# Two-pass products with v, a doubled output buffer and MLP groups dealt in halves in a fused attention and MLP kernel

## The chip, the cores and the metric

The kernel runs on one core of a Trainium2 chip. Its time is device microseconds for one execution of the whole program.

## What is computed

Four batches of 8 heads of causal (in blocks of 64) attention over 576 positions with head dimension 64, then an MLP (512 to 2048 to 512, leaky ReLU), then a routed mixture of eight experts. All in float32 precision: operands are split into a high part, which TensorE's fp32r format holds, and a low rest, and a product is made of high x high, high x low and low x high.

```python
    scores = scale * np.matmul(q, k.transpose(0, 1, 3, 2))
    mask = block_i >= block_j
    scores = np.where(mask, scores, -1000000000.0)
    scores = scores - np.max(scores, axis=-1, keepdims=True)
    attn = np.exp(scores)
    attn = attn / (np.sum(attn, axis=-1, keepdims=True) + 1e-09)
    return np.matmul(attn, v).astype(np.float32)
...
    h = x @ w_in
    g = np.maximum(0.01 * h, h)
    return (g @ w_out).astype(np.float32)
```

The experts come after everything that the change touches.

## The kernel before

Heads are worked in 16 pairs of two. A pair has nine units, numbered i = 0 to 8: rows of queries in tiles of 128, four for the even head (i = 0 to 3), one that holds the last 64 rows of both heads (i = 4, TAIL), four for the odd head (i = 5 to 8). Unit u = 9p + i goes through: scores on TensorE (line 1219), maximum on VectorE (955), exponential on ScalarE (812, with the row's sum), transposes of the probabilities on TensorE (1251) into one of two PSUM banks of ps_t, then high part pt_hi on ScalarE (822) and low part pt_lo on VectorE (963). All engines run the same loop over steps s = 0 to 155, each with its own lag and in strict order: in step s TensorE does scores(s + 2), transposes(s - 2), products with v by the table P_V, then MLP groups by the table FILL; VectorE does maximum(s), low_p(s - 3); ScalarE does high_p(s - 3), exponential(s), then copies of MLP results of step s - 1.

The product with v of a pair (p_v, 1265) accumulates both heads in one bank, ps_o: v stands between zero columns, so that the even head fills rows 0 to 63 and the odd one 64 to 127. Per head there are two kinds: half 0 (query columns 0 to 255; two tiles of keys, six products) and half 1 (columns 256 to 575; five tiles, fifteen products of 320, 192 and 64 columns, dealt as eight in step 3 or 5 and seven in step 4 or 6). VectorE copies each half out of PSUM once (copy_o, 983), GpSimd multiplies it with the spread inverse of the row sums (normalise, 657), and from it come xh and xl, the MLP's input. v is rounded to v_hi on ScalarE (high_v, 802) and v_lo is made on GpSimd (low_v, 647). The row sums get their epsilon and are inverted on VectorE (invert, 968), turned on TensorE (turn_inverse, 1291) into ps_o, copied and spread through DRAM by SyncE.

An MLP group (hidden, 1295) is twelve products of 384 columns into one bank (ps_h1), and ScalarE copies it out (copy_hidden, 835; line 839 issues it). There are 96, of which 64 are dealt into the steps by fill_steps (76): groups 0 to 15 over steps 50 to 83, 16 to 47 over 86 to 119, 48 to 56 over 122 to 143, each whole at the end of a step; from group 57 on there are two banks and one group a step. w_in's 16 pieces are rounded on ScalarE (high_w_in, 830) every second step from 42 and completed on GpSimd. After step 155 the rest of the MLP and the experts follow.

## Time and profile before

| | us |
|---|---|
| median of 3 runs | 856.89 (856.85 to 856.97) |
| the profiled execution | 856.37 |
| its span | 854.5 |
| TensorE / VectorE / ScalarE / GpSimd busy | 810.5 / 414.2 / 359.7 / 196.8 |
| mean granted TensorE clock | 0.98 of 2.4 GHz |

Busy time is a share of the span over stages of different kind. An instruction's duration on TensorE overlaps the next one's, so what it costs is read from start to start. "Idle before" in brackets is how long the engine had nothing running before an instruction, with what ended that. The granted clock is the mean of a stretch over two levels, 2.4 GHz (1.0) and 1.2 GHz (0.5).

### The profile page before, as it was taken

The numbers are of one execution on the slowest core, as the hardware profiler recorded it, in microseconds if no ns is written. First come the engines' busy times: TensorE is split into PE (matmuls) and PEld (weight loads), VectorE is DVE, ScalarE is ACT, GpSimd is POOL, SyncE is SP. The second block draws the span as 40 slices with busy tenths as digits, with TensorE's granted clock in tenths as the row PEclk, the third lists the DMA queues.
The fourth block names the chain that finished last, engine by engine and source line by source line (L and its number), as shares of the span: only waits on it lengthen the run. The fifth ranks groups of instructions, "written<-read, shape, count | busy, mean of one in ns | idle before, by whom it ended". The sixth has DMA issues, their size and how long they took to land.

```text
span 854.5 us, 14147 instructions
## 1 busy us (share of the span) xinstructions
PE 810.5 (95%) x4885; PEld 736.9 (86%) x4885; DVE 414.2 (48%) x835; ACT 359.7 (42%) x850; POOL 196.8 (23%) x226
## 2 busy tenths in 40 slices
PE   4889999999999999999999999999999589999999
PEld 3778899999999999899998888888888489888887
DVE  4777766664334456402335455555553232344464
ACT  4677767665445566423442222221221031333353
POOL 5354666433213224110010000000000141221221
PEclk9999799999999999999999999999999879999999
DMA  6444466744453343136666655655561137577740
GB/s 149 132 122 136 142 186 195 203 126 141 118 146 112 105 137 105 50 98 193 173 180 182 190 148 172 182 180 145 168 186 50 38 113 248 174 216 233 227 135 3
DMA packets 101545, 126.82 MB, mean 148 GB/s; under 512 B 15986, under 2 KB 62210, under 8 KB 101480
## 3 DMA queue, kind: packets, MB, share of 16 engines
q1 hardware_dynamic: 98392, 121.33, 48.3%
q0 software_dynamic: 2000, 3.77, 1.4%
q10 hardware_dynamic: 1088, 0.89, 0.5%
q8 instruction: 37, 0.61, 0.3%
q14 instruction: 28, 0.23, 0.1%
HBM read 92.58 MB, written 31.57 MB: 145 GB/s over the span
## 4 chain that ended last, share of the span: by engine, by line
PE 89%; DVE 4%; issue 3%; ACT 3%; DMA 1%; POOL 0%; SPq 0%; DVEq 0%; ACTq 0%; POOLq 0%
PE ps_hid L1431 11%; PE ps_o L1286 9%; PE ps_h L1310 8%; PE ps_x L1345 8%; PE ps_x L1347 8%; PE ps_h L1312 8%; PE ps_h L1311 8%; PE ps_x L1346 8%; PE ps_t L1262 4%; PE ps_y L1442 3%; PE ps_y L1443 3%; PE ps_y L1444 3%; PE ps_s L1247 2%; PE ps_s L1248 2%; PE ps_s L1237 1%
## 5 line engine op out<-in xcount | busy, mean ns | idle before, releaser
L966 DVE TENSOR_TENSOR pt_lo<-ps_t,pt_hi 128x512 fp32r<-128x512 f32 (+4 forms) x160 | 76.5, 486 | 147.1 <-ACT pt_hi L828 146.8
L1310 PE MATMUL ps_h<-xh,win_h 128*128 128x384 f32 x384 | 132.8, 346 | 1.3 <-ACT act L839 1.0
L1311 PE MATMUL ps_h<-xl,win_h 128*128 128x384 f32 x384 | 128.8, 335 | 0.0
L1312 PE MATMUL ps_h<-xh,win_l 128*128 128x384 f32 x384 | 128.7, 335 | 0.0
L1345 PE MATMUL ps_x<-wout_h,g_hi 128*128 128x512 f32 x288 | 116.3, 404 | 0.0
L1347 PE MATMUL ps_x<-wout_h,g_lo 128*128 128x512 f32 x288 | 112.9, 392 | 0.0
L1346 PE MATMUL ps_x<-wout_l,g_hi 128*128 128x512 f32 x288 | 112.1, 389 | 0.0
L1431 PEld LDWEIGHTS ps_hid<-rows_t,w_sb 128*128 128x128 f32 x768 | 89.5, 196 | 8.8 <-issue 8.4
L1431 PE MATMUL ps_hid<-rows_t,w_sb 128*128 128x128 f32 x768 | 91.0, 281 | 5.1 <-PE ps_y L1444 4.2
L839 ACT ACTIVATE act<-ps_h 128x384 f32<-128x384 f32 x96 | 47.1, 491 | 110.1 <-PE ps_h L1312 108.4
L819 ACT ACTIVATE prob<-ps_s,neg_max 128x128 f32<-128x128 f32 (+2 forms) x144 | 78.9, 548 | 25.7 <-DVE neg_max L960 25.2
L828 ACT ACTIVATE pt_hi<-ps_t 128x512 fp32r<-128x512 f32 (+4 forms) x160 | 67.6, 434 | 50.3 <-PE ps_o L1286 31.4
L643 POOL TENSOR_TENSOR k_st<-k_raw,k_st 64x576 fp32r<-64x576 f32 x32 | 45.9, 1433 | 161.6 <-DVE k_st L946 151.1
L1262 PE MATMUL ps_t<-ident,prob 128*128 128x128 f32 x384 | 70.5, 288 | 5.3 <-DVE pt_lo L966 5.3
L1310 PEld LDWEIGHTS ps_h<-xh,win_h 128*128 128x128 f32 x384 | 72.1, 188 | 3.8 <-ACT act L839 1.7
L1003 DVE TENSOR_TENSOR g_lo<-g_raw,g_hi 128x512 fp32r<-128x512 f32 x72 | 49.5, 687 | 52.2 <-ACT g_hi L849 52.2
L960 DVE TENSOR_REDUCE neg_max<-ps_s 128x1 f32<-128x128 f32 (+2 forms) x144 | 72.4, 503 | 0.6 <-PE ps_s L1248 0.5
L1286 PE MATMUL ps_o<-pt_hi,v_hi 128*128 128x320 f32 (+3 forms) x224 | 69.6, 311 | 2.7 <-DVE o_f L988 2.7
L1311 PEld LDWEIGHTS ps_h<-xl,win_h 128*128 128x128 f32 x384 | 72.2, 188 | 0.0
L1312 PEld LDWEIGHTS ps_h<-xh,win_l 128*128 128x128 f32 x384 | 72.1, 188 | 0.0
L1286 PE MATMUL ps_o<-pt_hi,v_lo 128*128 128x320 f32 (+3 forms) x224 | 68.6, 306 | 0.0
L1286 PE MATMUL ps_o<-pt_lo,v_hi 128*128 128x320 f32 (+3 forms) x224 | 66.1, 295 | 0.0
(154 smaller groups left out, 1422.3 us busy)
## 6 DMA issues: line engine op xcount, KB each, us to landing
w_sb<-in_w SPq DMA_DIRECT2D x64, 512.0 KB, 5.2
hidden<-act SPq DMA_DIRECT2D x96, 192.0 KB, 2.2
g_raw<-hidden SPq DMA_DIRECT2D x72, 256.0 KB, 4.5
k_raw<-in_k_t SPq DMA_DIRECT2D x62, 144.0 KB, 2.9
q_raw<-in_q_t SPq DMA_DIRECT2D x32, 144.0 KB, 2.9
x2rows<-x SPq DMA_DIRECT2D x18, 256.0 KB, 2.4
out<-x SPq DMA_DIRECT2D x18, 256.0 KB, 2.6
k<-k_st SPq DMA_DIRECT2D x31, 144.0 KB, 2.7
```

The costliest lines, as they stand in the source:

```text
L819: e.activation(prob_of(u), score_out(u), ACT.Exp, bias=neg_max[:, u % 4:u % 4 + 1], scale=1.0, accum_out=row_sum[p % 2][:, i:i + 1]).then_ ...
L960: e.tensor_reduce(out=neg_max[:, u % 4:u % 4 + 1], in_=src, axis=AX.XY if u % UNITS == TAIL else AX.X, op=ALU.max, negate=True).then_inc(s ...
L966: e.tensor_tensor(lo, src, hi.bitcast(F32), ALU.subtract).then_inc(s_ptlo, 1)
L1262: last = e.transpose(t_bank(u, P, P * kt, P * kt + P), tile[:, P * kt:P * kt + P], ident[:, :])
L1286: last = e.matmul(ps_o[:, a:a + cols], stat, (pt_hi, pt_lo, pt_hi)[j][0:kr, h, at:at + cols], start=h == 0 and n == 0, stop=h == 1 and n = ...
L1310: e.matmul(dst, win_h[:, f, kc, :], xh[slot][:, kc, :], start=kc == 0, stop=False)
L1311: e.matmul(dst, win_h[:, f, kc, :], xl[slot][:, kc, :], start=False, stop=False)
L1312: last = e.matmul(dst, win_l[:, f, kc, :], xh[slot][:, kc, :], start=False, stop=kc == KC - 1)
L1345: e.matmul(dst, hi, wout_h[:, f, :], start=f == 0, stop=False)
L1346: e.matmul(dst, hi, wout_l[:, f, :], start=False, stop=False)
L1347: last = e.matmul(dst, lo, wout_h[:, f, :], start=False, stop=f == FC - 1)
L1431: last = e.matmul(ps_hid[half][:, P * f - HALF * half:P * (f + 1) - HALF * half], w1_sb[i][:, c, P * f:P * f + P], rows_t[:, c, :], start= ...
```

## The change

- Products with v: the stationary operand now holds high and low part of v side by side (v_st, four slots), so one pass with pt_hi and one with pt_lo give high rows and low rows at once; each head has its own high and low rows. The last 64 keys take one pass: v is loaded twice, into both halves of the partitions, and pt_lo of these keys goes into the lower half of pt_hi's tile. Four products for half 0, nine for half 1, in steps 7, 1, 3, 5. Three rounds of the bank: both heads' half 0 side by side, then half 1 of each head.
- Getting them out: ScalarE copies the low rows (copy_low, 4 per pair, steps 2, 2, 4, 6), VectorE adds them to the high rows (add_o), o_f has two buffers.
- Moves: v's and w_in's rounding to VectorE, the epsilon to ScalarE; v's load to step 4; low_v, low_x, normalise, low_q and copy_inverse to other steps; the inverse is turned into a bank of the transposes.
- A third bank (the MLP's, ps_h1) for transposes up to unit 44.
- MLP groups are issued in two halves of six products. The deal goes by halves up to group 56; a result is copied in the step after its second half. By the formula steps 50 to 83 and 122 to 143 hold at most one half each, steps 86 to 119 one or two: both of one group in 86 to 93 and 103 to 110, and the second of one with the first of the next in 95 to 101 and 112 to 118.

The diff, cut:

```diff
 STEPS = N_UNITS + 12
-P_V = {8: (0, 0, 0, 6), 1: (1, 0, 0, 6), 3: (0, 1, 0, 8), 4: (0, 1, 8, 15), 5: (1, 1, 0, 8), 6: (1, 1, 8, 15)}
+P_V = {7: (0, 0), 1: (1, 0), 3: (0, 1), 5: (1, 1)}
+V_EVEN, V_EVEN_LOW, V_ODD_LOW, V_ODD = range(4)
+V_SLOTS = 4
 MASKED = -float(1 << 30)
...
     for g in range(N_ATT_HID):
-        if g < FC:
-            at[50 + 34 * g // FC].append(g)
-        elif g < 3 * FC:
-            at[86 + 34 * (g - FC) // (2 * FC)].append(g)
-        elif g < TWO_BANKS:
-            at[122 + 5 * (g - 3 * FC) // 2].append(g)
-        else:
-            at[N_UNITS + 5 + g - TWO_BANKS].append(g)
+        for part in range(2):
+            n = 2 * g + part
+            if g < FC:
+                s = 50 + 34 * n // (2 * FC)
+            elif g < 3 * FC:
+                s = 86 + 34 * (n - 2 * FC) // (4 * FC)
+            elif g < TWO_BANKS:
+                s = 122 + 22 * (n - 6 * FC) // (2 * (TWO_BANKS - 3 * FC))
+            else:
+                s = N_UNITS + 5 + g - TWO_BANKS
+            at[s].append((g, part))
     return at
+def filled_at(s):
...
+    return u % 3 if u < T3_UNITS else u % 2
+def t_before(u):
+    return next((v for v in range(u - 1, max(u - 4, -1), -1) if t_index(v) == t_index(u)), None)
...
-            c = BANK * (u % 2)
-            return ps_t[0:rows_, c + a:c + z]
+            n = t_index(u)
+            return ps_h1[0:rows_, a:z] if n == 2 else ps_t[0:rows_, BANK * n + a:BANK * n + z]
...
                 return views
             src = t_bank(u, P, 0, P * (qt + 1)).rearrange("p (k q) -> p k q", q=P)
             return [[src] + [t[:, h, PT_B:PT_W].rearrange("p (k c) -> p k c", k=4)[:, 0:qt + 1, P * (qt - 2):P * (qt - 1)]
                              for t in (pt_hi, pt_lo)]]
...
-                e.wait_ge(s_vlo, 2 * p)
+                e.wait_ge(s_vlo, p)
             e.dma_start(v_raw[:, 0:QT - 1, :],
                         v_r[b, 0:full, hp * P:(hp + 1) * P].rearrange("(t p) c -> p t c", p=P)).then_inc(s_v, 16)
...
+                e.dma_start(v_raw[half:half + D, QT - 1, :], v_r[b, full:S, hp * P:(hp + 1) * P]).then_inc(s_v, 16)
...
                         copy_k(2 * p + 2)
+                    if i == 4 and p + 1 < N_PAIRS:
+                        load_v(e, p + 1)
...
-                    e.tensor_tensor(v_lo[i][0:rows_, t0:t1, 0:3:2, :],
-                                    v_raw[0:rows_, t0:t1, :].rearrange("p t (g c) -> p t g c", g=2),
-                                    v_hi[i][0:rows_, t0:t1, 0:3:2, :].bitcast(F32), ALU.subtract).then_inc(s_vlo, 1)
+                e.wait_ge(*before[0])
+                e.wait_ge(s_vhi, p + 1)
+                before[0] = s_vlo, p + 1
+                e.tensor_tensor(v_st[i][:, :, V_EVEN_LOW:V_ODD_LOW + 1, :],
+                                v_raw[:, :, :].rearrange("p t (g c) -> p t g c", g=2),
+                                v_st[i][:, :, V_EVEN:V_ODD + 1:V_ODD - V_EVEN, :].bitcast(F32),
+                                ALU.subtract).then_inc(s_vlo, 1)
...
                     if i == 7:
                         low_k(2 * p + 3)
-                if i == 2 and 1 <= p < N_PAIRS:
+                if i == 7 and 1 <= p <= N_PAIRS:
+                    normalise(p - 1)
+                if i == 1 and p < N_PAIRS:
                     low_v(p)
-                if i == 8 and 1 <= p <= N_PAIRS:
-                    normalise(p - 1)
-                if i == 1 and 2 <= p <= N_PAIRS + 1:
+                if i == 2 and 2 <= p <= N_PAIRS + 1:
                     low_x(p - 2)
                 f, odd = divmod(s - 42, 2)
...
+                rs = row_sum[p % 2]
+                e.wait_ge(s_exp, UNITS * (p + 1))
+                e.activation(rs[:, :], rs[:, :], ACT.Copy, bias=1e-9).then_inc(s_eps, 1)
+            def copy_low(p, h, half):
+                n = product(p, h, half)
+                cols = B_COLS if half else A_COLS
+                own, low = head_rows(h)
+                e.wait_ge(s_pv, n + 2 - h if half == 0 else n + 1)
+                if n >= 2:
+                    e.wait_ge(s_of, n - 1)
+                at = A_COLS * h if half == 0 else 0
+                e.activation(o_low[own, 0:cols], ps_o[low, at:at + cols], ACT.Copy).then_inc(s_olow, 1)
...
                 for src, hi, _ in pt_views(u):
...
-                    if i == 8:
-                        high_v(p + 1)
                     if i == 7:
                         high_q(2 * p + 3)
+                if i == 8 and p < N_PAIRS:
+                    add_epsilon(p)
+                if 1 <= p <= N_PAIRS:
+                    if i == 2:
+                        copy_low(p - 1, 0, 0)
+                        copy_low(p - 1, 1, 0)
+                    if i == 4:
+                        copy_low(p - 1, 0, 1)
+                    if i == 6:
+                        copy_low(p - 1, 1, 1)
                 if i == 0 and 2 <= p <= N_PAIRS + 1:
                     high_x(p - 2)
...
-                e.wait_ge(s_exp, UNITS * (p + 1))
-                e.tensor_scalar(rs[:, :], rs[:, :], 1e-9, None, ALU.add).then_inc(s_eps, 1)
...
-                e.reciprocal(inv[:, :], rs[:, :]).then_inc(s_inv, 1)
...
+                e.tensor_copy(inv_t[:, :], t_bank(UNITS * (p + 1), UNITS, 2 * P, 3 * P)).then_inc(s_invt, 1)
...
                 a, z = ((0, A_COLS), (A_COLS, S))[half]
-                e.wait_ge(s_pv, 4 * p + 2 * half + 2)
-                if p >= 1:
-                    e.wait_ge(s_norm, p)
-                e.tensor_copy(o_f[:, a:z], ps_o[:, 0:z - a]).then_inc(s_of, 1)
+                own, _ = head_rows(h)
+                n = product(p, h, half)
+                e.wait_ge(s_olow, n + 2 - h if half == 0 else n + 1)
+                if p >= 2:
+                    e.wait_ge(s_norm, p - 1)
+                at = A_COLS * h if half == 0 else 0
+                e.tensor_tensor(o_f[p % 2][own, a:z], ps_o[own, at:at + z - a], o_low[own, 0:z - a], ALU.add).then_inc(s_of, 1)
+            def high_v(p):
+                e.wait_ge(s_v, 48 * (p + 1))
+                if p >= 2:
+                    e.wait_ge(s_pv, 4 * (p - 1))
+                e.tensor_copy(v_st[p % 2][:, :, V_EVEN:V_ODD + 1:V_ODD - V_EVEN, :],
+                              v_raw[:, :, :].rearrange("p t (g c) -> p t g c", g=2)).then_inc(s_vhi, 1)
+            def high_w_in(f):
+                e.wait_ge(s_stage[f % 2], 16 * (f // 2 + 1))
+                e.tensor_copy(win_h[:, f, :, :], w_stage[f % 2][:, :].rearrange("p (k c) -> p k c", k=KC)).then_inc(s_winh, 1)
             def low_w_out(f):
...
                     low_q(2 * p + 1)
                 if i == 0 and 1 <= p <= N_PAIRS:
                     invert(p - 1)
-                if i == 2 and 1 <= p <= N_PAIRS:
+                if i == 3 and 1 <= p <= N_PAIRS:
                     copy_inverse(p - 1)
-                    copy_o(p - 1, 0)
-                if i == 7 and 1 <= p <= N_PAIRS:
-                    copy_o(p - 1, 1)
+                if 1 <= p <= N_PAIRS:
+                    if i == 2:
+                        add_o(p - 1, 0, 0)
+                        add_o(p - 1, 1, 0)
+                    if i == 4:
+                        add_o(p - 1, 0, 1)
+                    if i == 6:
+                        add_o(p - 1, 1, 1)
+                if i == 0 and p < N_PAIRS:
+                    high_v(p)
+                f, odd = divmod(s - 42, 2)
+                if odd == 0 and 0 <= f < FC:
+                    high_w_in(f)
...
-                i = u % UNITS
+                v, i = t_before(u), u % UNITS
+                if v is not None:
+                    e.wait_ge(s_ptlo, split_done(v))
+                    if v >= UNITS and v % UNITS == 0:
+                        e.wait_ge(s_invt, v // UNITS)
...
+            def p_v(p, h, half):
+                n = product(p, h, half)
+                e.wait_ge(s_ptlo, split_done(UNITS * p + (1, TAIL + 1, TAIL + 2, UNITS - 1)[2 * h + half]))
+                if n % 4 == 0:
+                    e.wait_ge(s_vlo, p + 1)
+                if n % 4 != 1 and n >= 2:
+                    e.wait_ge(s_of, n)
+                at_o = A_COLS * h if half == 0 else 0
+                v = v_st[p % 2]
+                steps = [(kt, low) for kt in range(4 if half else 2) for low in range(2)]
+                if half:
+                    steps.append((QT - 1, 0))
+                for kt, low in steps:
...
+                last.then_inc(s_pv, 1)
...
                 slot = m % 4
+                dst = ps_hidden(g)
+                if part == 0:
+                    hidden_waits(g)
+                for kc in range(KC // 2 * part, KC // 2 * (part + 1)):
+                    e.matmul(dst, win_h[:, f, kc, :], xh[slot][:, kc, :], start=kc == 0, stop=False)
+                    e.matmul(dst, win_h[:, f, kc, :], xl[slot][:, kc, :], start=False, stop=False)
+                    last = e.matmul(dst, win_l[:, f, kc, :], xh[slot][:, kc, :], start=False, stop=kc == KC - 1)
+                if part:
+                    last.then_inc(s_h, 1)
+            def hidden_waits(g):
+                m, f = divmod(g, FC)
+                if g == 0:
+                    e.wait_ge(s_ptlo, split_done(T3_UNITS - 1))
                 if f == 0:
                     e.wait_ge(s_xlo, x_ready(m))
...
                     e.wait_ge(s_act, g)
-                dst = ps_hidden(g)
-                for kc in range(KC):
-                    e.matmul(dst, win_h[:, f, kc, :], xh[slot][:, kc, :], start=kc == 0, stop=False)
-                    e.matmul(dst, win_h[:, f, kc, :], xl[slot][:, kc, :], start=False, stop=False)
-                    last = e.matmul(dst, win_l[:, f, kc, :], xh[slot][:, kc, :], start=False, stop=kc == KC - 1)
-                last.then_inc(s_h, 1)
             scores(0)
             scores(1)
             for s in range(STEPS):
                 if s + 2 < N_UNITS:
                     scores(s + 2)
+                p, i = divmod(s, UNITS)
+                if i == 2 and 1 <= p <= N_PAIRS:
+                    turn_inverse(p - 1)
                 if 2 <= s < N_UNITS + 2:
                     transposes(s - 2)
...
+                for part in range(2):
+                    hidden(g, part)
```

## Rows read from the trace of the kernel before

**Rows 1.** The page, part 1: busy us, share of the span, instructions of each engine.
```profile
PE 810.5 (95%) x4885; PEld 736.9 (86%) x4885; DVE 414.2 (48%) x835; ACT 359.7 (42%) x850; POOL 196.8 (23%) x226
```

**Rows 2.** Busy time by stage: stretch, length, busy (instructions) of each engine, granted clock.
```profile
26.50:104.70 78.20, 68.62 (x422) 60.44 (x421) 57.57 (x128) 54.02 (x158) 39.46 (x35) 0.89 0.46 130
104.70:185.50 80.80, 80.24 (x542) 77.53 (x540) 50.04 (x108) 56.25 (x159) 45.84 (x39) 1.00 0.64 181
...
188.50:303.90 115.40, 114.67 (x732) 110.88 (x730) 49.29 (x107) 59.16 (x163) 29.44 (x27) 1.00 0.43 125
...
59.80:76.50 16.70, 14.91 (x95) 13.25 (x94) 12.44 (x28) 11.60 (x36) 7.63 (x8) 0.91 0.44 126
...
136.70:156.90 20.20, 20.20 (x139) 19.59 (x139) 12.98 (x28) 15.17 (x44) 13.44 (x11) 1.00 0.58 176
...
200.10:231.90 31.80, 31.62 (x203) 30.62 (x202) 12.83 (x28) 16.05 (x45) 7.71 (x7) 1.00 0.43 123
```

**Rows 3.** Timeline of TensorE in a filled pair: start us, duration us, engine, line, operation.
```profile
128.22 0.39 PE L1286 MATMUL ps_o<-pt_hi,v_hi 128*128 128x320 f32 x1
...
129.47 0.39 PE L1247 MATMUL ps_s<-k_st,q_hi 128*128 128x512 f32 x1
...
130.29 0.39 PE L1286 MATMUL ps_o<-pt_hi,v_lo 128*128 128x320 f32 x1
130.52 0.25 PE L1286 MATMUL ps_o<-pt_hi,v_hi 128*128 128x192 f32 x1
...
130.93 0.29 PE L1286 MATMUL ps_o<-pt_hi,v_hi 64*128 64x64 f32 x1
...
131.38 0.44 PE L1310 MATMUL ps_h<-xh,win_h 128*128 128x384 f32 x1
131.66 0.34 PE L1311 MATMUL ps_h<-xl,win_h 128*128 128x384 f32 x1
131.83 0.35 PE L1312 MATMUL ps_h<-xh,win_l 128*128 128x384 f32 x1
...
138.72 0.36 PE L1286 MATMUL ps_o<-pt_hi,v_hi 128*128 128x256 f32 x1
...
139.44 0.27 PE L1293 MATMUL ps_o<-ident,inv 128*9 128x128 f32 x1
```

**Rows 4.** The same timeline with ScalarE: one MLP group's end to the next one's start.
```profile
202.23 0.33 PE L1312 MATMUL ps_h<-xh,win_l 128*128 128x384 f32 x1
...
202.60 0.49 ACT L839 ACTIVATE act<-ps_h 128x384 f32<-128x384 f32 x1 [1.38 <-PE ps_h L1312]
...
203.14 0.44 PE L1310 MATMUL ps_h<-xh,win_h 128*128 128x384 f32 x1
```

**Rows 5.** Instructions by line: count, shortest, median and longest ns.
```profile
L988 DVE COPY o_f<-ps_o x32: 402/440/491, 31.0 to 366.9; 128x256 f32<-128x256 f32 x16, 128x320 f32<-128x320 f32 x16
...
L946 DVE CAST k_st<-k_raw x32: 437/450/1102, 7.8 to 333.7; 128x576 fp32r<-128x576 f32 x32
...
L971 DVE TENSOR_SCALAR row_sum<-row_sum x16: 156/764/979, 28.1 to 357.3; 128x9 f32<-128x9 f32 x16
...
L828 ACT ACTIVATE pt_hi<-ps_t x160: 258/428/604, 16.3 to 358.2; 128x512 fp32r<-128x512 f32 x48, 128x128 fp32r<-128x128 f32 x32, 128x256 fp32r<-128x256 f32 x32, 128x384 fp32r<-128x384 f32 x32
...
L808 ACT ACTIVATE v_hi<-v_raw x32: 293/462/627, 12.3 to 336.6; 128x512 fp32r<-128x512 f32 x16, 64x128 fp32r<-64x128 f32 x16
```

**Rows 6.** VectorE's timeline, 43 to 60 us, idle in brackets; and waits, 43.1 to 93.7.
```profile
51.95 0.56 DVE L966 TENSOR_TENSOR pt_lo<-ps_t,pt_hi 128x384 fp32r<-128x384 f32 x1 [0.86 <-ACT pt_hi L828]
...
56.03 0.69 DVE L966 TENSOR_TENSOR pt_lo<-ps_t,pt_hi 128x512 fp32r<-128x512 f32 x1 [1.40 <-ACT pt_hi L828]
...
59.92 0.42 DVE L966 TENSOR_TENSOR pt_lo<-ps_t,pt_hi 128x256 fp32r<-128x256 f32 x1 [1.25 <-ACT pt_hi L828]
...
PE ps_t L1262 <- DVE pt_lo L966: 3.0, 4, 0.8
```

**Rows 7.** Busy time by stage, the end of the stretch without filler, units 45 to 49.
```profile
93.70:104.70 11.00, 9.99 (x50) 8.93 (x49) 7.87 (x16) 7.20 (x22) 9.07 (x8) 0.62 0.39 120
```

107 lines of the change are left out of this document (34 added, 73 removed).

## The prediction

> **What bounds the kernel now.** I read the page first: TensorE is busy 95% of the span, VectorE 48%, ScalarE 42% [rows 1]. An average hides stages, so next came busy time by stage, cut where the exponentials (line 819, one per unit, nine units per pair of heads) of units 9, 50, 86, 120 and 143 start [rows 2]. Three kinds of stretch show. From 104.7 to 355.5 us MLP groups fill TensorE and it has 0.6 and 0.7 us idle in stages of 81 and 115 us: there every product less is time less. From 26.5 to 104.7 no MLP work exists, TensorE is idle 9.6 of 78.2 us, its granted clock averages 0.89, and no engine is full: waits between engines set the pace, 16.7 us a pair. Everything after 372 us is untouched. Last I read TensorE's timeline for what a product costs from start to start (durations overlap, so they overstate it) [rows 3, 4], and VectorE's waits in a pair without filler [rows 6].
>
> **1. Products with v.** Each head had 6 + 15 products and gets 4 + 9. Of the second kind, the first part of 8 took 129.47 - 128.22 = 1.25 us, the other 7 took 131.38 - 130.29 = 1.09. The first product after transposes costs 0.23 (130.29 to 130.52), each later one of 320 columns (1.25 - 0.23)/7 = 0.146; three of 192 stand between 130.52 and 130.93; the three with 64 rows take 0.45 [rows 3]. New: 0.23 + 5 x 0.146 + 0.20 (two of 192, a step of 0.1 each without the 64-row product behind them) + 0.11 (one of 64 columns, now over 128 rows: a little above the step of 192 columns, below the 0.15 of a 64-row one) = 1.27, so 2.34 - 1.27 = 1.07 saved. First kind: six took 139.44 - 138.72 = 0.72; 0.08 of it is the entry (0.23 - 0.146), and four of six leave 0.08 + 0.43 = 0.51, so 0.21 saved. Per head 1.28, **per pair 2.6 us**. Bounds for that 128-row product: 0.05 and 0.20, 0.2 us a pair at most.
>
> **2. Halving the MLP groups.** Two things follow from the new deal. (a) Entering a group costs 131.66 - 131.38 = 0.28 against 0.17 inside it (131.83 - 131.66) [rows 3]: 0.1 us per extra entry. Groups 0 to 15 and 48 to 56 are split over two steps: 25 extra entries, 2.5 us. (b) In steps 95 to 101 and 112 to 118 the formula puts the second half of group g and the first half of g + 1 in one step, 14 times. Both use one PSUM bank, so the later half waits until ScalarE has copied g. The trace has that handover at its shortest: last product starts 202.23, copy 202.60 to 203.09, next group's first product 203.14 [rows 4]. That is 0.91 against 0.17 back to back, **0.74 us** of idle TensorE; in the kernel before, scores and transposes lay in this gap, now nothing does. 14 x 0.74 = 10.4 us. ScalarE issues that copy after the next step's pt_hi, exponential and whatever else the step holds. Where that is a q_hi (0.6), a pair of xh (0.7) or two new copies (0.7), the copy comes some 0.5 us later: 7 of the 14 steps, 3.8 us with small change. Bounds of (b): 10.4 and 18.
>
> **3. Halves of the output.** Products leave high and low rows apart, so ScalarE copies one half (4 per pair) and VectorE adds (4 per pair, instead of 2 copies). No such form is in the trace; nearest are the copies of the same columns on VectorE, median 0.44, and ScalarE's pt_hi from PSUM, median 0.43 [rows 5]. Neighbouring instructions overlap by a little under 0.1, so 1.4 us more for ScalarE, 0.8 for VectorE per pair. Bounds per instruction 0.3 and 0.6. The adds stand in VectorE's queue in front of the next maximum, and behind a ScalarE copy: in step 2 TensorE's next product waits for exp, two copies and two adds, where it waited for two copies of VectorE. I take 0.9 us a pair for this where there is no filler, and nothing where TensorE lags behind the others anyway. Bounds 0 and 2.
>
> **4. Moves between engines.** v's rounding (two instructions of 0.29 to 0.63 on ScalarE) and w_in's (16 of about 0.6) go to VectorE, where a cast of 128x576 has a median of 0.45; the epsilon (median 0.76 on VectorE) goes to ScalarE, estimated at 0.2 from pt_hi's shortest, 0.26 [rows 5]. Per pair VectorE: -0.9 + 0.45 + 0.8 = +0.35, and 4.5 x 0.45 = 2.0 in the pairs with w_in; ScalarE: -0.7 + 0.15 + 1.4 = +0.85. In the shortest filled pair VectorE goes from 13.0 to 15.4 of then some 18 us, ScalarE stays at 15 or below [rows 2]: covered by TensorE, VectorE narrowly. The epsilon shows a danger: nine columns took from 0.16 to 0.98 us, and the cast reached 1.10 [rows 5]. The Trainium skill (SBUF — State Buffer, Who interferes with whom) says the same of such pairs: a VectorE copy in a two-port mode and a GpSimd instruction exclude each other for a whole instruction. The trace agrees in kind with the 0.98; by the rule each of the 32 new casts might gain that delay. A median close to the cast's shortest (0.45, 0.44) says that it is rare, and the sum goes by that.
> GpSimd: one v_lo instead of two, low x a step later (needed three steps later), normalising a step earlier; it is busy 13.4 of 20.2 us at most [rows 2]. SyncE: v's load moves from step 2 to 4 and gets a third DMA; behind it stand the spreading of the inverse at step 5 and the hidden stores; its wait (v_lo of step 1) has long been met. On ScalarE's queue the third DMA stands ahead of the first table load at the start, while four memsets leave GpSimd: I take 0, between -1 and +2 (two fewer or four more instructions of v_hi's 0.46 on that path). The turned inverse shares a transpose bank and holds the transposes of unit 2 until VectorE's step 3 ends: bounds 0 and 0.7 a pair without filler, in the value below.
>
> **5. The stretch without filler.** VectorE is busy 12.4 of 16.7 us and idles 4.3 [rows 2], 3.5 of it in three waits for pt_hi, 0.86, 1.40 and 1.25 us [rows 6]. The first two end when a product lump of step 4 or 6 is done, as its pt_hi may not overwrite what the product reads; the lumps now end in steps 3 and 5. The third follows v_hi (0.7) on ScalarE, now gone. The third bank takes TensorE's wait for pt_lo (3.0 us in three pairs) [rows 6]. So of 4.3 the three waits go but for 0.1, and 1.4 come (0.9 of point 3, 0.5 for the inverse and the later adds): 2.3 idle and 12.4 + 0.35 busy make 15.05, **1.65 saved a pair**. Bounds: no idle at all (12.7) and nothing saved.
>
> **The sum** against the profiled 856.4 (span 854.5 and 1.9 around it; the median of the runs is 0.5 higher):
> - 0 to 26.5: 0.
> - 26.5 to 104.7, 4.7 pairs: -7.8.
> - 104.7 to 185.5, units 50 to 83, 3.8 pairs: -9.8, +1.6 (16 entries), +1.5 (where the next half follows a short step, up to 0.3 of the 0.91 shows): -6.7.
> - 185.5 to 188.5, one product group: -1.
> - 188.5 to 303.9, 3.8 pairs: -9.8 + 10.4 + 3.8 = **+4.4**. This stage gets slower.
> - 303.9 to 355.5, 2.7 pairs: -7.0 + 0.9 + 0.7 = -5.4.
> - 355.5 to 372: -2.4, +0.9 for adds with nothing beside them: -1.5.
> Together -18.0: 838.4, as a median **838.9**.
>
> **Rivals.**
> A. *The halves cost nothing* (0.12): the bank handover is hidden and the second filled stage gives its 9.8. For it: in the kernel before nearly every copy lay beside other products. Against: the copy's end and the next product stand 0.05 apart [rows 4]. -18.0 - 14.2: 824.7.
> B. *The new copy and add bind* (0.12): without filler nothing is gained, and the first filled stage loses another 3 us as VectorE, with its w_in casts, makes TensorE wait. For it: VectorE has 50.0 of 80.8 us there already [rows 2], and waits stand in strict queues. Against: TensorE saturated. -18.0 + 7.8 + 3: 849.7.
> C. *TensorE's clock stays low* (0.06), the slower side. The granted clock is 0.89 over the stretch without filler [rows 2], a fifth of it at the lower level, and 0.62 over its end [rows 7]. Less product work makes the engine quieter. Its work in a pair: 31.8 us [rows 2] less 8.5 groups of 12 x 0.173 + 0.1 = 2.18 is 13.3, then 10.7. All at 1.2 GHz it is 21.4 instead of 16.7: +22 over 4.7 pairs, 838.9 + 7.8 + 22 = 869. It makes the whole slower once a pair takes 18.8, that is with three quarters of the stretch at the low level; now it is a fifth. Against: at the low level the same work keeps TensorE busy, and it came back each time. The Trainium skill (TensorE: Matmul & The Clock Gate, The HAM clock gate) has the same two levels and says that activity releases the throttle; it speaks for a swing, not for staying low.
>
> **How the numbers follow.** Forecast 0.70, A 0.12, B 0.12, C 0.06. The forecast's own range, from the bounds of points 2, 3 and 5 that don't all fall together, is 830 to 847; to hold 8 in 10 it is widened to 827 to 850, which takes in B and part of A's near side. This kernel's runs tell 0.2% (1.7 us) from no change. Faster: all but C and an edge of B, 0.92; same 0.02; slower 0.06.
>
> **What would show it.** Step 1: 416 products at ps_o instead of 672, starts 0.146 apart. Step 2: 14 idle times of 0.7 to 1.3 us before the first MLP product, ended by ScalarE's act, and units 86 to 119 taking 118 to 122 us instead of 115.4. Step 3: TensorE waiting for o_f in step 3 of pairs without filler. Step 5: 15 us between pairs' first exponentials. Wrong would be: units 86 to 119 below 112 us (A), pairs of 16.5 without filler (B), a clock below 0.75 before unit 50 (C).

## The result and the profile after

The changed kernel takes 865.1 us (median of 4 runs, 863.95 to 866.94) against 856.9 for the kernel before on the same chip: ratio 1.009, 95% interval 1.007 to 1.011. It is 0.9% slower, where 838.9 was forecast. Its profiled execution took 864.9 us, with a span of 863.1; the kernel before had 854.5.

The page of the changed kernel: busy time, share of the span and instructions of each engine, then the first product of the MLP groups (busy, mean ns, idle before it and what ended that).

```profile
PE 784.2 (91%) x4629; PEld 705.8 (82%) x4629; DVE 445.6 (52%) x883; ACT 370.9 (43%) x882; POOL 194.0 (22%) x206
...
L1357 PE MATMUL ps_h<-xh,win_h 128*128 128x384 f32 x384 | 137.8, 359 | 20.9 <-ACT act L866 20.6
```

TensorE has 256 matmuls fewer and 26.3 us less busy time than in [rows 1], and the kernel is 8.6 us longer: TensorE's idle time went from 44.0 to 78.9 us. Of that, 20.6 stand at the first product of an MLP group and wait for ScalarE's copy of the group before.

Busy time by stage (stretch, length, busy and instructions of TensorE, its weight loads, VectorE, ScalarE, GpSimd, then granted clock, DMA share, GB/s), cut where [rows 2] is cut; the second row ends 3.6 us before unit 86, and the last is one pair without filler:

```profile
25.90:109.70 83.80, 61.45 (x349) 53.46 (x347) 66.52 (x143) 58.58 (x168) 39.00 (x30) 0.84 0.45 126
109.70:190.20 80.50, 73.95 (x480) 69.90 (x481) 61.49 (x127) 55.15 (x157) 45.62 (x35) 1.00 0.65 181
...
193.80:313.00 119.20, 107.67 (x661) 100.52 (x662) 53.52 (x113) 62.13 (x171) 29.25 (x23) 1.00 0.44 121
313.00:361.80 48.80, 45.62 (x307) 43.42 (x306) 34.34 (x74) 35.52 (x102) 17.12 (x13) 1.00 0.39 106
361.80:388.30 26.50, 22.62 (x122) 22.00 (x121) 4.34 (x11) 8.51 (x21) 4.54 (x5) 0.87 0.20 62
...
78.50:97.20 18.70, 13.98 (x78) 12.65 (x77) 14.92 (x33) 12.96 (x39) 9.30 (x8) 0.78 0.53 150
```

Set against the forecast, with the stages named by the exponentials that bound them (us; "miss" is measured less forecast):

| stage | before | after | measured | forecast | miss |
|---|---|---|---|---|---|
| start to unit 9 | 26.5 | 25.9 | -0.6 | 0 | -0.6 |
| units 9 to 49, no filler | 78.2 | 83.8 | +5.6 | -7.8 | +13.4 |
| units 50 to 85 | 83.9 | 84.0 | +0.1 | -7.7 | +7.8 |
| units 86 to 119 | 115.3 | 119.3 | +4.0 | +4.4 | -0.4 |
| units 120 to 142 | 51.6 | 48.8 | -2.8 | -5.4 | +2.6 |
| 143 to the first MLP group after attention | 23.9 | 26.5 | +2.6 | -1.5 | +4.1 |
| the rest | 475.1 | 474.8 | -0.3 | 0 | -0.3 |

So the third row of loss was foreseen and the first, the largest, was not: half of the miss lies where there is no MLP work.

Next the waits of that stretch, 26 to 105 us of the kernel before and 26 to 110 of the changed one (engine, line, what it waited for: total us, times, longest). Before:

```profile
DVE pt_lo L966 <- ACT pt_hi L828: 20.1, 23, 1.8
...
PE ps_t L1262 <- DVE pt_lo L966: 4.0, 6, 0.8
...
PE ps_s L1237 <- ACT prob L819: 3.4, 5, 0.7
```

After:

```profile
PE ps_s L1288 <- DVE q L981: 13.5, 5, 2.7
DVE o_f L1018 <- ACT o_low L842: 10.7, 14, 1.0
...
DVE pt_lo L996 <- ACT pt_hi L860: 6.0, 13, 0.8
```

The waits that the forecast removed did go: VectorE's for pt_hi fell from 20.1 to 6.0 us, TensorE's for pt_lo is not in the list. In their place TensorE stands still once a pair, 2.7 us, before the scores of step 2 (line 1288), and VectorE waits at the adds. The timeline around one such place (start, duration, engine, line, operation, idle before it in brackets):

```profile
60.74 1.42 POOL L688 TENSOR_TENSOR inv_all<-o_f,inv_all 128x576 f32<-128x576 f32 x1
...
61.54 0.76 DVE L1024 CAST v_st<-v_raw 128x640 fp32r<-128x640 f32 x1
...
62.19 0.78 ACT L826 ACTIVATE xh<-inv_all 128x384 fp32r<-128x384 f32 x2 [0.80 <-POOL inv_all L688]
...
62.88 0.47 ACT L860 ACTIVATE pt_hi<-ps_t 128x384 fp32r<-128x384 f32 x1
...
63.38 0.56 DVE L996 TENSOR_TENSOR pt_lo<-ps_t,pt_hi 128x384 fp32r<-128x384 f32 x1 [0.75 <-ACT pt_hi L860]
...
63.85 0.81 DVE L981 SCALAR_TENSOR_TENSOR q<-q_raw,q_hi 64x640 fp32r<-64x640 f32 x1
...
64.91 1.18 PE L1288 MATMUL ps_s<-k_st,q_hi 128*128 128x288 f32 x4 [2.68 <-DVE q L981]
```

Read backwards: the scores wait for q, q stands in VectorE's queue behind pt_lo, pt_lo waits for pt_hi, pt_hi stands in ScalarE's queue behind xh, and xh waits for GpSimd's normalise. VectorE's own casts stand in the same chain. Which link carries the time a timeline can't say; the experiments had to.

### The profile page after: what moved, and what is told of

The parts are those of the page before. It is cut to its first block, busy times and chain, and to the rows that moved or that the text cites. A ratio compares the mean times of both kernels' runs of the same rounds, so it can differ in the third digit from the quotient of the medians.

```text
span 863.1 us, 13813 instructions
## 1 busy us (share of the span) xinstructions
PE 784.2 (91%) x4629; PEld 705.8 (82%) x4629; DVE 445.6 (52%) x883; ACT 370.9 (43%) x882; POOL 194.0 (22%) x206
## 4 chain that ended last, share of the span: by engine, by line
PE 76%; ACT 7%; issue 6%; DVE 6%; POOL 2%; DMA 1%; SPq 1%; ACTq 1%; DVEq 0%; POOLq 0%
PE ps_hid L1495 10%; PE ps_x L1409 8%; PE ps_x L1411 8%; PE ps_x L1410 8%; PE ps_h L1357 7%; PE ps_h L1359 6%; PE ps_h L1358 6%; PE ps_o L1339 3%; PE ps_t L1315 3%; PE ps_y L1506 3%; PE ps_y L1507 3%; PE ps_y L1508 3%; ACT prob L851 2%; DVE neg_max L990 2%; DVE q L981 2%
## 5 line engine op out<-in xcount | busy, mean ns | idle before, releaser
L1357 PE MATMUL ps_h<-xh,win_h 128*128 128x384 f32 x384 | 137.8, 359 | 20.9 <-ACT act L866 20.6
L996 DVE TENSOR_TENSOR pt_lo<-ps_t,pt_hi 128x128 fp32r<-128x128 f32 (+2 forms) x129 | 65.8, 510 | 90.4 <-ACT pt_hi L860 89.7
L860 ACT ACTIVATE pt_hi<-ps_t 128x512 fp32r<-128x512 f32 (+4 forms) x140 | 60.0, 437 | 62.4 <-PE ps_t L1315 61.7
L670 POOL TENSOR_TENSOR k_st<-k_raw,k_st 64x576 fp32r<-64x576 f32 x32 | 46.3, 1446 | 162.5 <-DVE k_st L976 162.5
L1339 PE MATMUL ps_o<-pt_hi,v_st 128*128 128x320 f32 (+3 forms) x224 | 65.3, 310 | 5.4 <-DVE o_f L1018 5.3
L876 ACT ACTIVATE g_hi<-g_raw 128x512 fp32r<-128x512 f32 x72 | 43.6, 627 | 50.6 <-DVE g_raw L1039 42.7
L1298 PE MATMUL ps_s<-k_st,q_hi 128*128 128x128 f32 (+3 forms) x128 | 47.2, 369 | 18.7 <-POOL ident L708 10.6
L1411 PEld LDWEIGHTS ps_x<-wout_h,g_lo 128*128 128x128 f32 x288 | 54.0, 188 | 12.1
```

What stands on the lines that cost most here:

```text
L860: e.activation(hi, src, ACT.Copy).then_inc(s_pthi, 1)
L996: e.tensor_tensor(lo, src, hi.bitcast(F32), ALU.subtract).then_inc(s_ptlo, 1)
L1339: last = e.matmul(ps_o[:, at_o + a:at_o + a + cols], v[:, kt, 2 * h:2 * h + 2, :].rearrange("p g c -> p (g c)"), (pt_lo if low else pt_hi) ...
L1357: e.matmul(dst, win_h[:, f, kc, :], xh[slot][:, kc, :], start=kc == 0, stop=False)
L1411: last = e.matmul(dst, lo, wout_h[:, f, :], start=False, stop=f == FC - 1)
```

## The experiments

Stage lengths of all of them (us, same marks; the last column is the median with the ratio to the kernel before on the same chip). Each profile is one execution; a step under about 1 us is not read. The ratio is to the kernel before in the same set of runs, whose median was 856.9 in the first and 858.5 to 859.4 in the later ones, so medians of different sets differ by up to 2 us for that alone.

| kernel | 9 to 49 | 50 to 85 | 86 to 119 | 120 to 142 | median, ratio |
|---|---|---|---|---|---|
| before | 78.2 | 83.9 | 115.3 | 51.6 | 856.9 |
| after | 83.8 | 84.0 | 119.3 | 48.8 | 865.1, 1.009 |
| e1 | 82.3 | 82.8 | 119.3 | 48.8 | 862.9, 1.005 |
| e2 | 84.0 | 84.2 | 106.0 | 48.5 | 851.3, 0.991 |
| e3 | 78.1 | 89.8 | 127.7 | 56.6 | 881.7, 1.027 |
| e4 | 82.0 | 80.5 | 106.0 | 46.2 | 845.0, 0.984 |
| e5 | 79.9 | 81.5 | 106.0 | 46.7 | 844.2, 0.982 |
| e6 | 80.3 | 79.3 | 106.0 | 46.7 | 841.8, 0.979 |
| e7 | 76.7 | 77.3 | 106.6 | 44.5 | 835.0, 0.972 |
| e8 | 81.9 | 81.0 | 106.0 | 46.2 | 845.1, 0.983 |
| e9 | 83.6 | 80.4 | 106.0 | 47.3 | 847.2, 0.988 |
| e10 | 80.0 | 80.9 | 106.1 | 46.6 | 841.4, 0.980 |
| e11 | 84.2 | 81.1 | 106.0 | 47.7 | 845.2, 0.984 |
| e12 | 84.3 | 85.9 | 113.1 | 49.7 | 862.1, 1.006 |
| e13 | 74.1 | 77.4 | 106.6 | 46.4 | 833.3, 0.971 |
| e14 | 78.4 | 78.5 | 106.3 | 46.3 | 837.6, 0.976 |

**e1: the second low_q back in step 0.** The wait in the timeline above names q, and the change moved it a step later.

```diff
-                if i == 1 and 1 <= p < N_PAIRS:
+                if i == 0 and 1 <= p < N_PAIRS:
                     low_q(2 * p + 1)
```

> The changed kernel with one line moved back: VectorE's low part of the odd head's q is made in step 0 again, ahead of the inverse and of v's rounding, instead of at the end of step 1. Theory 1 (TensorE's wait of 2.7 us per pair before the scores of unit 4 is the wait for this instruction, and it also brings the clock down): pairs without filler fall from 17.5 to about 15.5 us, units 9 to 49 from 83.8 to about 74 us, the whole to about 854. Rival (the same engine has the same work, so the wait only moves to the maxima and exponentials behind it): pairs stay within 0.5 us of 17.5, the whole within 2 us of 865.

Measured 862.9 us, the stage 82.3: 1.5 us of 5.6. Most of the wait is still there, 10.7 of 13.5 us over the stretch, under another name; around one place:

```profile
59.93 1.43 POOL L688 TENSOR_TENSOR inv_all<-o_f,inv_all 128x576 f32<-128x576 f32 x1
...
60.60 1.43 DVE L981 SCALAR_TENSOR_TENSOR q<-q_raw,q_hi 64x640 fp32r<-64x640 f32 x1
...
62.08 0.75 DVE L1024 CAST v_st<-v_raw 128x640 fp32r<-128x640 f32 x1
62.76 0.40 DVE L990 TENSOR_REDUCE neg_max<-ps_s 128x1 f32<-128x256 f32 x1
...
63.20 0.47 ACT L851 ACTIVATE prob<-ps_s,neg_max 128x256 f32<-128x256 f32 x1 [0.66 <-DVE neg_max L990]
...
63.91 1.20 PE L1288 MATMUL ps_s<-k_st,q_hi 128*128 128x288 f32 x4 [2.48 <-ACT prob L851]
```

The scores of step 2 take two of the ring's four banks at once; they now wait for the exponential that frees the second, it for the maximum, and that for v's cast and for q, which beside GpSimd's normalise took 1.43 us instead of 0.81. The move alone is a small part of the loss.

**e2: MLP groups of units 86 to 119 whole again.**

```diff
             elif g < 3 * FC:
-                s = 86 + 34 * (n - 2 * FC) // (4 * FC)
+                s = 86 + 34 * (g - FC) // (2 * FC)
```

> The changed kernel with groups 16 to 47 dealt whole again, one per step, so that no step holds the second half of one group and the first of the next; all else as changed. Theory (each of the 14 handovers of the bank costs TensorE 0.74 us and more): units 86 to 119 fall from 119.3 to about 105 us and the whole to about 851. Rival A (the handovers are covered, TensorE is short of other things): less than 4 us.

Measured 851.3 us. The stage falls from 119.3 to 106.0 us and TensorE is busy 105.5 of it; no other stage moves by more than 0.3. The waits at a group's first product, in this stage of the changed kernel and of e2:

```profile
PEld ps_h L1357 <- ACT act L866: 16.6, 17, 1.5
...
PE ps_h L1357 <- ACT act L866: 11.2, 14, 1.2
```

```profile
PEld ps_h L1357 <- ACT act L866: 1.9, 6, 0.4
```

Fourteen waits of the product: the number of shared steps is the one that the formula gives. They are 11.2 us of idle time, 0.80 each; TensorE's busy time in the stage is 2.2 us longer as well (107.7 against 105.5). Together that is 13.3 us, 0.95 for each place, between the two bounds of the forecast.

**e3: the kernel before with its MLP groups in halves, and nothing else.** Its deal is the changed kernel's, with twice as many issues of six products.

```diff
-                for g in FILL[s]:
-                    hidden(g)
+                for g, part in FILL[s]:
+                    hidden(g, part)
```

> The kernel before with the changed kernel's deal of half groups and nothing else. Theory: 14 x 0.74 to 1.0 = 10 to 14 us more in units 86 to 119 (115.3 to 126 or above), 0.1 us for each of 25 more entries elsewhere, the whole 868 to 874. Rival (the deal in halves smooths the steps and gains where a whole group made engines wait): units 50 to 85 and 120 to 142 get shorter by more than 1 us each.

Measured 881.7 us, 1.027 of the kernel before, above the 868 to 874 that were expected. Nothing changes before unit 50; then +5.9, +12.4 and +5.0 us. In units 50 to 85 no step holds parts of two groups. TensorE is busy 84.2 of 89.8 us there, where the kernel before had 83.3 of 83.9: 5.0 of the 5.9 us are idle time. That is 0.37 for each of the 16 groups split. The waits of that stage:

```profile
PEld ps_h L1310 <- issue: 5.5, 5, 1.7
PE ps_h L1310 <- ACT act L847: 4.5, 4, 1.5
...
PE ps_h L1310 <- POOL win_l L684: 1.0, 1, 1.0
```

Five waits of 5.5 us carry it, four of them for the copy. The second half of one group stands at the end of its step and the first half of the next in the following one; where little lies between, the bank is not free. Halves cost in all three filled stages, and the forecast had seen nearly all of the price in the middle one.

**e4: both together (q's step and whole groups everywhere).** The rest of the change stays.

```diff
-                s = 50 + 34 * n // (2 * FC)
+                s = 50 + 34 * g // FC
...
-                s = 122 + 22 * (n - 6 * FC) // (2 * (TWO_BANKS - 3 * FC))
+                s = 122 + 5 * (g - 3 * FC) // 2
```

> The changed kernel with low q back in step 0 and all groups dealt whole, as in the kernel before. If the two causes are separate, the gains add: units 9 to 49 about 74 us, units 86 to 119 about 105 us, the whole about 838 to 842. If VectorE and ScalarE then bind in units 50 to 85, that stage stays at 80 us or above and the whole near 845.

Measured 845.0 us, 0.984. Against the kernel before, the middle stage gives 9.3 us, close to the 9.8 of point 1; but units 50 to 85 give 3.4 instead of 9.8, and the stretch without filler still loses 3.8. It is the base of what follows.

**e12: the products' work as before, on e4's base.** Three passes instead of two and three of the last keys' part, pt_hi's pass counted twice.

```diff
-                steps = [(kt, low) for kt in range(4 if half else 2) for low in range(2)]
+                steps = [(kt, low) for kt in range(4 if half else 2) for low in (0, 1, 0)]
                 if half:
-                    steps.append((QT - 1, 0))
+                    steps += [(QT - 1, 0)] * 3
```

> As the kernel with low q in step 0 and whole groups (844.95 us), with the products with v issued three times per tile as in the kernel before (21 per head instead of 13; the output is not right, one pass is counted twice). It shows where the saved products count. Theory: in the filled stages their whole time, 3.8 x 2.5 = 9.5 us in units 86 to 119 and less in 50 to 85, where VectorE binds; in the stretch without filler nothing to 1 us a pair, because no chain there runs through them. Rival (they count everywhere): units 9 to 49 up by 4.7 x 2.5 = 12 us.

Measured 862.1 us. It puts back 7.1 us in units 86 to 119 (the other 2.2 of e4's 9.3 come with the rest of the change, such as fewer pieces of a product and the last keys over 128 rows, which no run parts), 5.4 in units 50 to 85, and only 2.3 in the stretch without filler, 0.5 a pair. By the middle stage's price, 7.1 over 3.8 pairs, it would be 8.8: where there is no filler, three quarters of the products' work lies beside waits. This splits the stretch's balance: the rest of the change costs 84.3 - 78.2 = 6.1 us there, the products return 2.3. In units 50 to 85 the rest costs 2.0 (85.9 against 83.9).

**e5 and e6: the roundings back on ScalarE**, v's first, then w_in's too (two functions moved, on e4).

```diff
-                if i == 0 and p < N_PAIRS:
-                    high_v(p)
...
+                if i == 8 and p + 1 < N_PAIRS:
+                    high_v(p + 1)
...
+                e.activation(v_st[p % 2][:, :, V_EVEN:V_ODD + 1:V_ODD - V_EVEN, :],
+                             v_raw[:, :, :].rearrange("p t (g c) -> p t g c", g=2), ACT.Copy).then_inc(s_vhi, 1)
```

> As the kernel with low q in step 0 and whole groups (844.95 us), with v's rounding back on ScalarE at the end of step 8 instead of VectorE's step 0. Theory 2 (without filler the chain runs through VectorE's steps 0 and 1: q, inverse, v's rounding, maximum, then ScalarE's exponential and the scores of unit 4): 0.5 to 0.7 us of the chain goes, pairs without filler fall from 17.3 to 16.6 us or below, units 9 to 49 from 82.0 to about 79 us, the whole to about 841. Rival (ScalarE gets the same delay in the same place, in front of the same exponential): no change within 1 us.

> The same with w_in's rounding back on ScalarE too. Theory 3 (in units 50 to 85 VectorE, busy 64 of 80.5 us, binds instead of TensorE): 16 instructions of 0.45 us leave it and that stage falls from 80.5 to 76 or 77 us, what TensorE's saved products would give; the whole to about 837. Rival (ScalarE becomes the bound there): 79 us or more.

Measured 844.2 and 841.8 us. Both expectations asked for more, 841 and 837. v's rounding is worth 2.1 us in the stretch without filler, of which 1.0 is lost again in units 50 to 85, and the intervals of e4's and e5's ratios overlap; w_in's is worth 2.2 in units 50 to 85. VectorE's busy time in the stretch fell by 6.4 us (68.3 to 62.0) for 1.7 us of time: its load alone does not set the pace. ScalarE took the work over, so this does not say what less work would bring.

**e7: no low rows.** The copies of the low rows are left out and the adds are copies of the high rows of the same size, so the output lacks the low rows' part.

```diff
-                e.wait_ge(s_olow, n + 2 - h if half == 0 else n + 1)
+                e.wait_ge(s_pv, n + 2 - h if half == 0 else n + 1)
...
-                e.tensor_tensor(o_f[p % 2][own, a:z], ps_o[own, at:at + z - a], o_low[own, 0:z - a], ALU.add).then_inc(s_of, 1)
+                e.tensor_copy(o_f[p % 2][own, a:z], ps_o[own, at:at + z - a]).then_inc(s_of, 1)
```

> As the kernel with low q in step 0 and whole groups (844.95 us), but the low rows are left out: ScalarE doesn't copy them and VectorE copies the high rows alone, four times per pair, so the part of the output from v's low rows is missing. It prices the handover from TensorE by ScalarE to VectorE. Theory 4 (VectorE's queue stands at each add until ScalarE has copied, 8 us in units 9 to 49, and the products of the next step wait for the add): units 9 to 49 fall from 82.0 to about 75 us, units 50 to 85 from 80.5 to about 77, the whole to about 833. Rival (the waits are slack): less than 2 us in either stage.

Measured 835.0 us: -5.3 in the stretch, -3.2 in units 50 to 85. The handover from ScalarE to VectorE is the largest single part found. The two stages, e4 and then e7:

```profile
25.80:107.80 82.00, 62.89 (x349) 55.74 (x348) 68.34 (x143) 58.77 (x168) 38.20 (x30) 0.79 0.46 129
107.80:188.30 80.50, 75.48 (x497) 71.54 (x497) 64.12 (x133) 58.08 (x164) 47.20 (x36) 1.00 0.66 188
```

```profile
26.00:102.70 76.70, 60.24 (x343) 54.30 (x342) 67.83 (x142) 50.50 (x149) 37.37 (x30) 0.80 0.48 134
102.70:180.10 77.40, 74.62 (x498) 71.52 (x499) 62.67 (x132) 51.71 (x150) 47.69 (x37) 1.00 0.69 197
```

VectorE has as much to do as in e4, and ScalarE 8.3 us less in the first stage. The gain is that of ScalarE's copies and of VectorE standing still for them; this run can't part the two.

**e8: two banks for the transposes**, as before.

```diff
-T3_UNITS = 5 * UNITS
+T3_UNITS = 0
```

> As the kernel with low q in step 0 and whole groups (844.95 us), with two banks for the transposes throughout instead of three up to unit 44. If the third bank carries something, the 1 us per pair that transposes waited for pt_lo before comes back: units 9 to 49 from 82.0 to 84 or 86 us. If VectorE and ScalarE set the pace there, no more than 1 us.

Measured 845.1 us against 845.0, the stretch 81.9 against 82.0. The third bank is worth nothing on this base.

**e9: GpSimd normalises before it takes the low part of k**, on e6's base. The timeline of after shows xh waiting 0.80 us for the normalise.

```diff
-                    if i == 7:
-                        low_k(2 * p + 3)
                 if i == 7 and 1 <= p <= N_PAIRS:
                     normalise(p - 1)
+                if p + 1 < N_PAIRS:
+                    if i == 7:
+                        low_k(2 * p + 3)
```

> As the kernel with low q in step 0, whole groups and both roundings on ScalarE (841.75 us), with GpSimd's step 7 turned round: it normalises first and makes the low part of k after it. Theory 5 (there the chain of a pair without filler runs k's cast, low k, normalise, xh, pt_hi: GpSimd's two instructions of 1.4 us stand in it one behind the other, while GpSimd idled 6 us before): pairs without filler fall from 16.9 to about 15.5 us, units 9 to 49 from 80.3 to 74 us, the whole to about 835. Rival (the adds and exponentials set the same pace by themselves): less than 2 us.

Measured 847.2 us against e6's 841.8, the stretch 83.6 against 80.3. The theory falls. There was little left to gain: in e6 the waits of xh for the normalise are 0.5 us over the stretch, none above 0.2, where the changed kernel has 3.0. And the multiply now begins beside VectorE's cast of k, and that cast took 1.67 us for a median of 0.45. The low part of k begins at 60.40, later by the multiply's 1.41 us and by 0.46 more for the cast; which of the two costs the 3.3 us no run parts:

```profile
58.53 1.41 POOL L688 TENSOR_TENSOR inv_all<-o_f,inv_all 128x576 f32<-128x576 f32 x1 [5.65 <-DMA inv_all<-inverse]
...
58.58 1.67 DVE L996 CAST k_st<-k_raw 128x576 fp32r<-128x576 f32 x1
...
60.40 1.40 POOL L670 TENSOR_TENSOR k_st<-k_raw,k_st 64x576 fp32r<-64x576 f32 x1 [0.46 <-DVE k_st L996]
```

**e10: TensorE's idle time filled** with products that nobody reads, two transpose banks, on e6's base.

```diff
+                if 9 <= s < 50:
+                    for _ in range({7: 2, 8: 4, 0: 4, 1: 4}.get(i, 0)):
+                        e.matmul(ps_h1[:, 0:P], ident[:, :], ident[:, :], start=True, stop=True)
```

> As the kernel with low q in step 0, whole groups and both roundings on ScalarE (841.75 us), with two transpose banks and with products that nobody reads in TensorE's quiet steps 7, 8, 0 and 1 of the stretch without filler (14 per pair, of 128 float32 columns, into the free bank). Theory 6 (the clock at the lower level for 6.8 of 17 us a pair, which doubles the 1.3 us that the scores of unit 4 take, costs about 1 us per pair): granted clock of that stretch from 0.82 to 0.95 or above, pairs shorter by 0.7 to 1.5 us, the whole 836 to 839. Rival (the low clock only costs where TensorE would wait anyway, and the added products delay scores): no gain, or up to 1 us a pair more.

Measured 841.4 us against 841.8. The granted clock from 43 to 94 us, e6 and then e10 (the column behind the busy times):

```profile
43.00:94.00 51.00, 41.88 (x229) 36.71 (x230) 39.83 (x87) 41.65 (x117) 24.76 (x20) 0.80 0.48 133
```

```profile
43.00:94.00 51.00, 43.61 (x317) 37.85 (x316) 39.72 (x89) 41.52 (x117) 25.07 (x20) 1.00 0.47 136
```

The mean is 1.00, the level of 2.4 GHz, where e6 has parts at 1.2, and the stretch is as long as it was, 80.0 against 80.3. The scores of step 2 were not the place: in e6 they take 0.76 to 0.78 us in four of five pairs, as in e10, and the lower level follows behind them (0.50 from 64.4 to 71.2 us, TensorE busy 6.3 of 6.8). On this base the low clock costs nothing that the time shows. The changed kernel itself, whose scores of step 2 take up to 1.30 us, was not tried, and the added products may have eaten a small gain. TensorE's waits stand elsewhere now; the largest is for the adds, 2.1 us in e6:

```profile
PE ps_o L1342 <- DVE o_f L1037: 7.3, 9, 1.1
```

**e11: e9 and e10 together**, to see whether the normalise's order pays once the clock is up.

> Normalising first and the idle steps filled, both on the same base (841.75 us). If both causes are real and separate: pairs without filler at 14.5 to 15 us and the whole at 831 to 834. If they are the same microseconds: no better than the better of the two alone.

Measured 845.2 us, the stretch 84.2, no better than e9 alone. It doesn't.

**e13: e6 and e7 together**, roundings on ScalarE and no low rows (the output again lacks their part).

> As the kernel with low q in step 0, whole groups and both roundings on ScalarE (841.75 us), with the low rows left out (neither copied by ScalarE nor added by VectorE, which copies the high rows alone, so the part of the output from v's low rows is missing). If the handover and the roundings are separate costs, units 9 to 49 fall from 80.3 to about 75 us, below the 78.2 of the kernel before, and the whole to about 832. If one only covers the other, that stage stays at 76.7 us or above, as with the low rows left out and the roundings on VectorE.

Measured 833.3 us; the stretch is 74.1, 15.8 us a pair. Against e6 that is 6.2 us less. So even without ScalarE's copies and the wait for them only 4.1 us of the stretch are gained, where the forecast had 7.8 with the handover paid.

**e14: the adds right behind the maximum**, on e6's base. Each add moves from the end of VectorE's step 2, 4 or 6 to the middle of the next step; ScalarE's copy then has a maximum's time to land.

```diff
                     maximum(s)
+                if 1 <= p <= N_PAIRS:
+                    if i == 3:
+                        add_o(p - 1, 0, 0)
+                        add_o(p - 1, 1, 0)
+                    if i == 5:
+                        add_o(p - 1, 0, 1)
+                    if i == 7:
+                        add_o(p - 1, 1, 1)
```

> As the kernel with low q in step 0, whole groups and both roundings on ScalarE (841.75 us), with VectorE's adds issued one step later, behind the next step's maximum. The work is the same; only VectorE no longer stands still until ScalarE has copied (8.1 us of such waits in the four pairs from 26 to 95 us). If the waiting is the cost: units 9 to 49 fall from 80.3 to 77 us or below, units 50 to 85 from 79.3 to about 78, the whole to about 837. If it is the added work, or TensorE's wait for the later add takes its place: within 1 us of 841.75, or above.

Measured 837.6 us, 0.976 [0.974 to 0.979], less than both kernels and e6: its median is 4.2 lower, its span 3.5 (837.0 against 840.5), with the same instructions. By the ratios it is 2.5 us and the intervals overlap (e6: 0.978 to 0.981), so that it is faster than e6 rests on the waits, and the size is uncertain. In the stretch, e6 and then e14:

```profile
ACT prob L863 <- DVE neg_max L1009: 10.7, 13, 1.8
DVE o_f L1037 <- ACT o_low L854: 9.5, 14, 0.9
DVE pt_lo L1015 <- ACT pt_hi L872: 8.4, 12, 1.7
```

```profile
DVE pt_lo L1015 <- ACT pt_hi L872: 11.9, 16, 1.7
...
ACT prob L863 <- DVE neg_max L1009: 6.6, 11, 1.8
...
DVE o_f L1037 <- ACT o_low L854: 5.0, 8, 1.0
```

The exponential waits 4.1 us less for the maximum, VectorE 4.5 less for the copy, and the stretch is 1.9 us shorter. VectorE hardly idles less, 17.9 us for 18.3, as it waits 3.5 more for pt_hi: what counts is that the maximum is no longer behind the wait. An instruction that stands at a semaphore in an in-order queue makes all that is behind it late.

## Why the prediction was wrong

**Point 1, the products: right in TensorE's work, wrong in how much of it counts.** 416 products at ps_o as forecast, 0.145 us apart, and 0.09 to 0.12 for the narrow ones; the nine of half 1 take 223.27 - 222.06 = 1.21 us, forecast 1.27:

```profile
222.06 0.39 PE L1339 MATMUL ps_o<-pt_hi,v_st 128*128 128x320 f32 x1
222.28 0.31 PE L1339 MATMUL ps_o<-pt_lo,v_st 128*128 128x320 f32 x1
...
223.01 0.25 PE L1339 MATMUL ps_o<-pt_hi,v_st 128*128 128x192 f32 x1
...
223.22 0.22 PE L1339 MATMUL ps_o<-pt_hi,v_st 128*128 128x64 f32 x1
223.27 0.42 PE L1357 MATMUL ps_h<-xh,win_h 128*128 128x384 f32 x1
```

Where TensorE is full the kernel gains 9.3 us (e4) for a forecast of 9.8, 7.1 of them by the number of products (e12). Without filler it is 2.3 for some 8.8 of work (e12).

**Point 2, the halves: (b) right, (a) too small.** The stage of units 86 to 119 was forecast at 119.8 and took 119.3, with 14 places that cost 0.95 us each (e2) for 0.74 plus 0.27. Seven of the 14 waits are 0.58 us and seven 0.79 to 1.21, the two kinds that the forecast named. The entries of the other stages were put at 0.1 us, and 1.5 us for the handover to the next step; e3 shows 5.9 against 3.1 in units 50 to 85, and 5.0 against 1.6 in units 120 to 142. On the changed kernel itself undoing them gives 2.3 and 2.6 (e4 less e1, since e4 also moves q's step, worth 1.2 us in units 50 to 85). The mis-sized term is the handover between steps: the forecast gave it "up to 0.3" where a wait reaches 1.5.

**Point 5, the stretch without filler: the failed step.** 15.05 us a pair were forecast, 17.5 came, 18.7 in the last. The step said that of VectorE's 4.3 idle us a pair three waits go and 1.4 us come, and that 0.35 is added to its busy time. The first half held: VectorE's waits for pt_hi fell by 14.1 us. But 10.7 came at the adds alone, and VectorE's idle time over the stretch fell only from 78.2 - 57.6 = 20.6 us to 83.8 - 66.5 = 17.3, where the forecast leaves 4.7 x 2.3 = 10.8. And its busy time rose by 8.9 us, 1.9 a pair: 4.7 by adds in place of copies, 3.8 by v's casts, 1.9 by w_in's, 0.9 by longer instructions for q, less 4.3 for the epsilon, and the rest by less overlap. v's cast of 640 columns took 0.76 us and not the 0.45 of k's 576, and w_in's four casts, which point 4 names, are not in this stretch's sum. So the miss is about half idle time (6.5 us) and half busy time (7.3) of VectorE. The busy time alone is no cause: e6 takes 6.4 us of it away for 1.7. In pieces of the stretch, by the runs:

| from the kernel before | us |
|---|---|
| e13: products, bank, moves, handover without low rows | -4.1 |
| + low rows copied and added (e6 less e13) | +6.2 |
| + v's and w_in's rounding on VectorE (e4 less e6) | +1.7 |
| + low_q a step later (after less e4) | +1.8 |
| after | +5.6 |

For what e13 runs, the forecast amounts to 14.1 us saved: 7.8, the handover's idle time 4.7 x 0.9 = 4.2, and v's rounding 4.7 x 0.45 = 2.1. Measured are 4.1, so 10.0 of the 13.4 us missed here lie in what is left without low rows and casts:

```profile
26.40:100.50 74.10, 60.37 (x341) 53.73 (x339) 60.62 (x133) 55.02 (x158) 39.24 (x30) 0.82 0.50 140
```

VectorE idles 74.1 - 60.6 = 13.5 us in e13, 2.9 a pair, where the forecast without the handover's 0.9 leaves 1.4. So by VectorE's account an estimated 7 of the 10 us are idle time that was counted as gone with its three waits. The handover adds 2.0 (6.2 against 4.2), low_q 1.8, and the roundings take 0.4 off (1.7 against 2.1). Emptying a wait in this ring of VectorE, ScalarE and TensorE brought only what the next wait in it left over; the third bank, credited with 3.0 us of waits, brought nothing (e8). What remains late in e13 is not settled. Its largest wait of TensorE in the stretch is the same place, the scores of step 2:

```profile
PE ps_s L1272 <- ACT prob L852: 7.4, 5, 2.1
```

In the kernel before that wait was 3.4 us. e1 and e5 each moved a suspect out of its chain without removing it (10.7 and 5.6 us left), and what no run tried is another order of ScalarE's step 0, where pt_hi stands behind xh.

**Point 3, the handover: the right mechanism, the wrong price.** 0.9 us a pair was taken from bounds of 0 and 2; e13 against e6 gives 1.3 (with ScalarE's copies gone too, so it is a price of copies and wait together). "Nothing where TensorE lags behind the others" is where it failed more: units 50 to 85 lose 3.2 us to it (e7), or 1.9 with the roundings on ScalarE (e13 against e6). **Point 4:** v's and w_in's casts were put under TensorE's cover, VectorE "narrowly". They cost 1.2 us there (e6). The cover is the same in both: once point 1 takes 9.8 us from TensorE in this stage, it is no longer the last; it is busy 75.5 of e4's 80.5 us. I subtracted the whole saving and kept the cover that it uses up.

**The drain (143 to the MLP's own groups):** +2.6 for -1.5. The changed kernel's three waits in it are 0.94 for pt_lo, 1.67 and 1.13 for the adds:

```profile
367.19 0.38 PE L1339 MATMUL ps_o<-pt_hi,v_st 128*128 128x320 f32 x1 [1.67 <-DVE o_f L1018]
...
369.70 0.61 PE L1339 MATMUL ps_o<-pt_hi,v_st 128*128 128x320 f32 x1 [1.13 <-DVE o_f L1018]
```

```profile
368.80:375.70 6.90, 6.00 (x21) 6.03 (x22) 0.98 (x2) 0.66 (x2) 1.42 (x1) 0.51 0.14 43
```

With one bank in three rounds, a head's half 1 can't begin until the round before is copied and added; the kernel before had one such wait, 1.27. Behind it the clock granted is 0.51, its lower level, for 6.9 us in which TensorE is busy 6.0 of them; before it was 1.00 throughout. Here, unlike in e10, TensorE has the work that all wait for. No run parts the two, but the rows give an estimate: TensorE idles 26.5 - 22.6 = 3.9 us in the drain for 2.1 before, 1.8 more; and in those 6.9 us the products of 320 columns start 0.27 us apart instead of 0.145, so that 6.0 busy us would be some 3.2 at the upper level, 2.8 more. The forecast had 0.9 for the adds and nothing for the clock.

**The rivals.** A fell (the handover of the bank costs 13.3 us). B was the nearest in mechanism: copies and adds that bind where there is no filler and in units 50 to 85 are what happened, with e7's 5.3 and 3.2 us. Its price of 10.8 us was too low as it let the stretch without filler break even, and it went only with its own term beyond the forecast, not with the halves' second price. C had the sign and, at 869, the nearest number, by luck: the clock over the stretch is 0.84, not 0.5, and e10 at 1.00 is no faster than its base. The Trainium skill (TensorE: Matmul & The Clock Gate, The HAM clock gate) says that activity releases the throttle; e10's 1.00 agrees. The rule of the Trainium skill (SBUF — State Buffer, Who interferes with whom) that the forecast set aside as rare was rare for the new casts: none of v's 16 took more than 0.80 us for a median of 0.76, and w_in's 0.71 at most for 0.42 (1.60 in e4). It shows through other instructions, q in e1 and k's cast in e9 (below).

## What to carry to other kernels

A wait read from a trace was here no measure of what its removal brings, and where several engines hand work round in strict order, several waits did not add up (14.1 us of waits went, 3.3 us of idle time): before summing them, ask for each what is late next. When a saving is subtracted from an engine that covers others, subtract the cover too, stage by stage. If a change adds a handover between engines, put the receiving instruction where its input is already there (e14, by its two measures 2.5 to 4.2 us, near the noise), and do not split an accumulation so that its last part meets the next one's first part in one bank (13.3 us here, more than all the products save in that stage).

## What the runs showed of the chip

- Two VectorE instructions beside a GpSimd multiply of 128x576 ended about as if they had begun when the multiply ended: q took 1.43 us for 0.81 (e1; multiply to 61.36, q to 62.03), a cast 1.67 for 0.45 (e9; 59.94 and 60.25). The Trainium skill (SBUF — State Buffer, Who interferes with whom) states it for casts in a two-port mode and for a VectorE instruction with two inputs from SBUF beside a GpSimd one that reads SBUF; both agree. Not every cast was held: v's, of 128x640, took 0.76 us beside this multiply (61.54 in the timeline of after) as it did alone.
- The clock fell to its lower level at times where TensorE stood idle often, and raising it brought nothing there (e6 and e10: 0.80 and 1.00, 80.3 and 80.0 us); in the drain of the changed kernel it fell with TensorE at work right behind two waits.
- A bank's handover from TensorE to ScalarE's copy and back, with nothing else to do, was a wait of 0.80 us on average (14 of them, 0.58 to 1.21) and cost 0.95 by e2, near the 0.91 less 0.17 of [rows 4] plus what stood in ScalarE's queue.
- The last 64 keys' part over 128 rows took 0.05 us from start to start (223.27 - 223.22), below the step of a 192-column product (0.09 and 0.12), where one over 64 rows had 0.15 [rows 3].
